# The first tile of a fused attention and MLP kernel in two units of 256 columns, with a rewritten prologue

## The reference

```
k_n = k / (norm(k) + 1e-6)
for t in range(768):
    y[t] = q[t] @ state
    v_old = state.T @ k_n[t]
    state = state + beta[t] * outer(k_n[t], v[t] - v_old)
x = y as (3072, 384)
h = maximum(x @ w_in, 0);  x = (h * h) @ w_out             # w_in 384 x 2048
g = x @ w_gate;  out = (silu(g) * (x @ w_val)) @ w_out2     # 384 x 1536
```

## Time and profile before

| | |
|---|---|
| time, median of 3 runs | 1124.94 us (1123.85 to 1128.55) |
| time of the profiled execution | 1125.86 us |
| its span, first to last instruction | 1124.1 us |
| PE busy | 1002.7 us (89%), 10464 matmuls |
| PE weight loads | 819.2 us (73%) |
| DVE, ACT, POOL busy | 422.8, 289.1, 243.1 us |
| mean granted TensorE clock | 0.983 |
| DMA | 73.83 MB, mean 66 GB/s |

### The profile page before, as it was taken

How to read it: one execution, slowest core, us unless ns; L and a number is a source line. 1 busy time by engine, 2 the same in 40 slices (tenths; PEclk the granted TensorE clock), 3 DMA queues, 4 the chain that set the end, 5 groups by cost and what they waited for, 6 DMA issues and landing times.

```text
span 1124.1 us, 23446 instructions
## 1 busy us (share of the span) xinstructions
PE 1002.7 (89%) x10464; PEld 819.2 (73%) x10464; DVE 422.8 (38%) x662; ACT 289.1 (26%) x553; POOL 243.1 (22%) x351
## 2 busy tenths in 40 slices
PE   2006869979999999999999989999999999999998
PEld 2005747858777777788788868888888888888886
DVE  1562527425354454444425651222222322221322
ACT  2101323313223232223234531121121211211211
POOL 1107706924932860780000000000000000000000
PEclk9999979989999999999999999999999999999999
DMA  7323264143125224213004400010010010100000
GB/s 247 98 76 105 89 181 134 34 118 120 53 56 163 67 71 133 68 36 99 21 2 153 155 29 29 1 57 1 1 57 1 1 57 1 57 1 1 29 1 28
DMA packets 74356, 73.83 MB, mean 66 GB/s; under 512 B 53136, under 2 KB 53264, under 8 KB 74256
## 3 DMA queue, kind: packets, MB, share of 16 engines
q1 hardware_dynamic: 71952, 66.04, 19.8%
q10 hardware_dynamic: 2304, 6.29, 1.6%
HBM read 56.59 MB, written 15.73 MB: 64 GB/s over the span
## 4 chain that ended last, share of the span: by engine, by line
PE 81%; DVE 5%; POOL 5%; DMA 4%; issue 2%; SPq 2%; ACT 1%; DVEq 0%; ACTq 0%; POOLq 0%
PE bank L770 81%; POOL tinv L297 2%; POOL prod L294 2%; DMA k_sq<-in_ky 1%; DMA inv_scratch<-tinv 1%; DVE tinv L297 1%; DVE prod L294 1%; DMA k_prep<-in_kt 1%; SPq L345 1%; PE bank L895 1%; SPq L375 1%; ACT gram L531 1%; DVE h_lo L731 1%; DVE stage L726 0%; DMA inv<-inv_scratch 0%
## 5 line engine op out<-in xcount | busy, mean ns | idle before, releaser
L770 PE MATMUL bank<-x_hi,w_hi 128*128 128x512 f32 x720 | 287.7, 400 | 5.0 <-DVE x_lo L744 3.8
L770 PE MATMUL bank<-x_lo,w_hi 128*128 128x512 f32 x720 | 283.9, 394 | 0.0
L770 PE MATMUL bank<-x_hi,w_lo 128*128 128x512 f32 x720 | 283.5, 394 | 0.0
L770 PE MATMUL bank<-h_hi,w_hi 128*128 128x512 f32 x504 | 202.8, 402 | 1.3 <-DVE h_lo L731 1.3
L770 PE MATMUL bank<-h_lo,w_hi 128*128 128x512 f32 x504 | 196.7, 390 | 0.0
L770 PE MATMUL bank<-h_hi,w_lo 128*128 128x512 f32 x504 | 196.4, 390 | 0.0
L754 DVE TENSOR_TENSOR stage<-bank,stage 128x512 f32<-128x512 f32 x72 | 49.8, 691 | 322.7 <-ACT stage L625 322.7
L770 PEld LDWEIGHTS bank<-x_hi,w_hi 128*128 128x128 f32 x720 | 137.1, 190 | 35.5 <-DVE x_lo L744 4.2
L770 PEld LDWEIGHTS bank<-x_hi,w_lo 128*128 128x128 f32 x720 | 137.3, 191 | 29.2
L770 PEld LDWEIGHTS bank<-x_lo,w_hi 128*128 128x128 f32 x720 | 137.3, 191 | 27.7
L726 DVE TENSOR_TENSOR stage<-stage 128x512 f32<-128x512 f32 x96 | 79.2, 825 | 181.8 <-ACT stage L601 181.6
(11 more groups left out here) (75 smaller groups left out, 604.2 us busy)
## 6 DMA issues: line engine op xcount, KB each, us to landing
w_raw<-in_w SPq DMA_DIRECT2D x12, 576.0 KB, 3.8
k_dim<-in_kt SPq DMA_DIRECT2D x12, 512.0 KB, 4.0
q_dim<-in_qt SPq DMA_DIRECT2D x12, 512.0 KB, 3.6
x1s<-in_w ACTq DMA_DIRECT2D x16, 384.0 KB, 4.0
k_prep<-in_kt SPq DMA_DIRECT2D x11, 512.0 KB, 4.5
k_sq<-in_ky SPq DMA_DIRECT2D x12, 384.0 KB, 3.6
v_tok<-in_vy SPq DMA_DIRECT2D x12, 384.0 KB, 3.6
x_scratch<-x1s SPq DMA_DIRECT2D x18, 256.0 KB, 2.6
```

The costliest lines, as they stand in the source:

```text
L770: return pe.matmul(dst, lhsT, rhs, start=start, stop=stop, **kw)
```

## The change

**Units.** The first MLP's six tiles become seven units (`UNITS`): tile 0 is run as two units of 256 columns, each with all 16 weight blocks, and tiles 1 to 5 as before. Unit 0 needs only chunk 0, so the chain of chunk 1 moves out of the prologue into unit 0, with chunk 2's; chunk 3 is in unit 1. Stages get new slots in all units (`G` at 0 and 10, `lane` at 16).

**Prologue.** Each engine gets a list of its own (`PE_FIRST`, `ACT_FIRST`, `DVE_FIRST`). PE's stages take turns over all eight banks. ACT issues half of tile 0's triangle stores and half of the exchange of its inverses, DVE takes the second bank of `G` 0 and 1, `U` 0, `Z` 0 and `Y` 0 (`SHARED`). `lane` 0 and `solve` 0 stand ahead of the norms of chunks 1 and later; four more staging buffers (`w1_spare`, in memory that `x_hi` and its neighbours use later) hold weight blocks 3 to 6.

**Substitution.** `solve` starts from the factors on the diagonal instead of from ones, so the multiplication of the whole block at its end is gone; the zeroing stands ahead of it. DVE's first block has tiles of its own.

**Elsewhere.** The squares of the keys go from POOL to ACT (`sq`). DVE's square reads relu from `stage` and the product from the PSUM bank, so PE waits for `square_done` instead of `relu_done` before it refills the bank. ACT takes one of the three copies at a unit's end. The split of the second MLP's first input moves ahead of the last nine down matmuls, and the tables for Sqrt and Silu are loaded ahead.

```diff
-    SUB = 2 * (HALF - 1) + 4
+    SUB = 2 * (HALF - 1) + 2
+    UNITS = [(0, 0, T // 2), (0, T // 2, T // 2)] + [(c, 0, T) for c in range(1, NIT)]
...
-        PROLOGUE = [("G", 0), ("root", 0), ("G", 1), ("QK", 0), ("scale", 0), ("G", 2), ("root", 1), ("G", 3),
-                    ("root", 2), ("root", 3), ("w1", 0), ("w1", 1), ("lane", 0), ("solve", 0), ("w1", 2), ("w1", 3),
-                    ("w1", 4), ("U", 0), ("Z", 0), ("lane", 1), ("DZ", 0), ("DS", 0), ("Y", 0), ("scale", 1),
-                    ("KS", 1), ("QK", 1), ("U", 1), ("Z", 1), ("DZ", 1), ("w1", 5), ("Y", 1), ("scale", 2),
-                    ("X", 0, 0), ("X", 0, 1), ("X", 0, 2), ("X", 0, 3)]
-        FIRST_PIECES = 6
+        PE_FIRST = [("G", 0), ("G", 1), ("G", 2), ("G", 3), ("QK", 0), ("U", 0), ("Z", 0), ("DZ", 0), ("Y", 0),
+                    ("DS", 0), ("X", 0, 0), ("X", 0, 1)]
+        ACT_FIRST = [("sq", 0), ("G", 0), ("tri", 0), ("G", 1), ("tri", 1), ("fetch", 1), ("fetch", 2), ("fetch", 3),
+                     ("root", 0), ("w1", 0), ("sq", 1), ("lane", 0), ("fetch", 4), ("fetch", 5), ("fetch", 6),
+                     ("G", 2), ("G", 3), ("w1", 1), ("w1", 2), ("w1", 3), ("w1", 4), ("w1", 5), ("w1", 6), ("fetch", 7),
+                     ("lane", 1), ("inv", 0), ("root", 1), ("U", 0), ("fetch", 8), ("Z", 0), ("sq", 2), ("Y", 0),
+                     ("X", 0, 0), ("X", 0, 1)]
+        DVE_FIRST = [("G", 0), ("root", 0), ("G", 1), ("w1", 0), ("lane", 0), ("solve", 0), ("lane", 1), ("scale", 0),
+                     ("root", 1), ("QK", 0), ("w1", 1), ("U", 0), ("w1", 2), ("w1", 3), ("Z", 0), ("w1", 4), ("DZ", 0),
+                     ("w1", 5), ("Y", 0), ("w1", 6), ("DS", 0), ("X", 0, 0), ("X", 0, 1)]
+        SHARED = [("G", 0), ("G", 1), ("U", 0), ("Z", 0), ("Y", 0)]
...
+            if u == 0:
+                for f, slot in zip(range(7, NF1), (0, 2, 4, 7, 9, 12, 14, 17, 19)):
+                    put(slot, "w1", f)
+                put(1, "scale", 1)
+                put(3, "KS", 1)
+                put(5, "QK", 1)
+                put(6, "U", 1)
+                put(8, "root", 2)
+                put(9, "Z", 1)
+                put(12, "DZ", 1)
+                put(12, "sq", 3)
+                put(15, "Y", 1)
+                put(16, "G", 4)
+                put(17, "root", 3)
+                put(18, "DS", 1)
+                put(20, "X", 0, 2)
+                put(21, "X", 0, 3)
+                put(22, "scale", 2)
+                put(23, "G", 5)
+                put(24, "KS", 2)
+                put(25, "sq", 4)
+                put(26, "QK", 2)
+                put(28, "U", 2)
+                put(29, "lane", 2)
+                put(30, "Z", 2)
+                put(31, "root", 4)
+                put(32, "DZ", 2)
+            elif u == 1:
...
-                for f in range(NF1 - FIRST_PIECES):
-                    put(2 * f + 1, "w1", FIRST_PIECES + f)
-            if c == NIT - 1:
-                for f in range(NF2):
-                    put(2 * f + 3, "w2", f)
+                t, p = u, u + 1
+                n0, n1, p0, p1 = 2 * t, 2 * t + 1, 2 * p, 2 * p + 1
+                if t < NIT:
+                    if p < NIT:
+                        put(0, "G", p0)
+                        put(10, "G", p1)
+                        put(16, "lane", p)
+                    put(2, "sq", n1)
+                    put(4, "root", n1)
+                    put(8, "scale", n1)
+                    chain(n0, dict(KS=2, QK=4, U=5, Z=7, DZ=9, Y=11, DS=12))
+                    chain(n1, dict(KS=14, QK=15, U=17, Z=19, DZ=21, Y=23, DS=24))
...
+        BANKS, BEFORE, holder = {}, {}, {}
+        def take(stage_, numbers):
+            BANKS[stage_] = [banks[b] for b in numbers]
+            BEFORE[stage_] = {holder[b] for b in numbers if b in holder}
+            for b in numbers:
+                holder[b] = stage_
+        turn = 0
+        for one in PE_FIRST:
+            count = 1 if one[0] == "X" else 2
+            take(one, [(5 + turn + i) % 8 for i in range(count)])
+            turn += count
+        FFN_AFTER = {b: holder[b] for b in range(5) if b in holder}
+        turn = 0
...
+        def w1_place(i):
+            if i < RING:
+                return x1s[:, i, :], w1_loaded[i], 1
+            if i < RING + SPARE:
+                return w1_spare[:, i - RING, :], w1_loaded[i], 1
+            k = i - RING - SPARE
+            return x1s[:, k % RING, :], w1_loaded[k % RING], 2 + k // RING
...
+        def solve(eng, t, a, x, products, steps, at):
...
-            then(eng.tensor_tensor(tri[:, :, :], tri[:, :, :], lane_nw[:, :].unsqueeze(1).to_broadcast([P, HALF, HALF]),
+            then(eng.tensor_tensor(a[:, :, :], a[:, :, :], lane_nw[:, :].unsqueeze(1).to_broadcast([P, HALF, HALF]),
                                    ALU.mult))
-            if t > 0:
-                eng.wait_ge(inv_stored, 16 * t)
-            then(eng.memset(tinv[:, :, :], 0.0))
-            then(eng.memset(tinv[:, :, :].rearrange("p s t -> p (s t)")[:, 0:HALF * HALF:HALF + 1], 1.0))
+            then(eng.tensor_copy(diagonal(x), lane_w[:, :]))
             for j in range(HALF - 1):
                 block = [P, j + 1, HALF - 1 - j]
-                share = prod[:, 0:block[1] * block[2]].rearrange("p (c i) -> p c i", i=block[2])
-                then(eng.tensor_tensor(share, tri[:, j:j + 1, j + 1:HALF].to_broadcast(block),
-                                       tinv[:, 0:j + 1, j:j + 1].to_broadcast(block), ALU.mult))
-                below = tinv[:, 0:j + 1, j + 1:HALF]
+                share = products[:, 0:block[1] * block[2]].rearrange("p (c i) -> p c i", i=block[2])
+                then(eng.tensor_tensor(share, a[:, j:j + 1, j + 1:HALF].to_broadcast(block),
+                                       x[:, 0:j + 1, j:j + 1].to_broadcast(block), ALU.mult))
+                below = x[:, 0:j + 1, j + 1:HALF]
                 then(eng.tensor_tensor(below, below, share, ALU.add))
-            then(eng.tensor_tensor(tinv[:, :, :], tinv[:, :, :], lane_w[:, :].unsqueeze(2).to_broadcast([P, HALF, HALF]),
-                                   ALU.mult))
...
+        def first_exchange(eng, i):
+            at = slice(lanes(0, i), lanes(0, i) + HALF)
+            eng.wait_ge(dve_sub_step, SUB)
+            eng.dma_start(inv_dram[0, at, :], first_tinv[at, :, :].rearrange("p s t -> p (s t)")
+                          ).then_inc(first_stored[i], 16)
+            eng.wait_ge(inv_zeroed, 2)
+            eng.wait_ge(first_stored[i], 16)
+            load_blocks(eng, 0, 0, i)
...
             load_k(0)
-            load_prep(1)
             load_ky(0)
-            load_q(0)
-            load_v(0)
             sp.dma_start(beta_sb[:, :, :], beta).then_inc(beta_loaded, 16)
+            store_triangles(sp, 0, 0)
+            store_triangles(sp, 1, 0)
+            load_triangles(0)
             load_prep(2)
-            store_triangles(0)
-            store_triangles(1)
-            load_triangles(0)
-            load_ktok(0)
-            load_k(1)
             load_ky(1)
             load_prep(3)
-            store_triangles(2)
+            load_v(0)
+            load_q(0)
+            load_ktok(0)
+            store_both(2)
+            store_both(3)
+            load_triangles(1)
+            load_prep(4)
+            load_k(1)
+            first_exchange(sp, 0)
...
+            pool.wait_ge(dve_sub_step, SUB)
+            for t in range(1, NIT):
+                if t > 1:
+                    pool.wait_ge(inv_stored, 16 * (t - 1))
+                pool.memset(tinv[:, :, :], 0.0).then_inc(tinv_zeroed, 1)
+                pool.wait_ge(tinv_zeroed, t)
+                solve(pool, t, tri, tinv, prod, sub_step, SUB * (t - 1))
...
-                        slot = stage[:, f % 2, :]
-                        dve.tensor_tensor(slot, slot, slot, ALU.mult).then_inc(square_done, 1)
-                    for stage_ in PLAN[c].get(2 * f, []):
+                        dve.tensor_tensor(stage[:, f % 2, 0:w], stage[:, f % 2, 0:w], up_bank[f % 2][:, 0:w], ALU.mult
+                                          ).then_inc(square_done, 1)
...
-            for c in range(NIT):
-                pe.wait_ge(x_ready, 4 * (c + 1))
+            for u, (c, c0, w) in enumerate(UNITS):
+                at = slice(c0, c0 + w)
+                pe.wait_ge(x_ready, 2 if u == 0 else 4 * (c + 1))
                 for f in range(NF1 + 2):
-                    i = NF1 * c + f
+                    i = NF1 * u + f
                     if f < NF1:
-                        if c == 0:
+                        if u == 0:
                             pe.wait_ge(w1_lo_done, f + 1)
+                        if f < 2:
+                            bank_free(u, f, f)
                         if i >= 2:
-                            pe.wait_ge(relu_done, i - 1)
+                            pe.wait_ge(square_done, i - 1)
                         for kc in range(KC):
                             cols = slice(kc * P, (kc + 1) * P)
```

469 lines of the change are left out of this document (252 added, 217 removed).

## The result

The changed kernel takes 1082.95 us (median of 4 runs, 1082.27 to 1083.66), the kernel before 1125.12 us (4 runs, 1123.85 to 1128.55). The ratio is 0.9614, with a 95% interval of 0.9594 to 0.9633: 42 us faster, where 69 were predicted.

What follows compares the result with a forecast made beforehand. PE was taken as the bound from tile 2 on. Gains of 46.3 (through the short units), 16.7 (tiles 1 to 3) and 6.2 (end) sum to 69.2 off 1125.9; less 0.9 for the median: 1056 us, range 1044 to 1078.

Steps and rivals of the forecast that it cites:

- The start of the substitution: Prologue: an earlier reload of the triangles lets `lane_t` run at 23.2 instead of 44.94, the block done at 49.8.
- From the inverse to the MLP: Prologue: `U` 0 at 56.2, then 15.2 us of stages; the MLP starts at 71.4 instead of 121.3, 49.9 us earlier.
- Unit 0 and 1: The two short units against tile 0: 112 us with stalls, so the middle tiles start at 183.4, 46.3 us earlier.
- the rival of the weight load as a bound: Short units: 256-column matmuls follow after 0.23 us instead of 0.12, giving 1117, or 0.19, giving 1096; chance 0.06.
- I add 7.5 (between 0 and 15): Short units: us added to 104.5 for PE's waits on DVE, ACT and weights and some time at 1.2 GHz.
- Tiles 1 to 3: 90.5 us per tile without stalls; tile 1 gains 11.9, tiles 2 and 3 2.4 each, 16.7 us together.
- The balance "56.3 against 55.9": Middle tiles: 56.3 us of work for the inverse against 55.9 of PE work until `U`; called even, no stall counted.
- The rival of late inverses: Inverses come late in units 2, 3 and 4, 7 us each, giving 1077; chance 0.17.
- The end: Start of the second MLP: the 3.78 us wait and twelve matmuls at 0.43 instead of 0.23 go, 6.2 us gained.
- Edits costed at nothing: Long units: the square from PSUM, ACT's copy and the keys' squares on ACT lie beside PE and cost nothing.

Runs made afterwards that it cites:

- final: lane_first with `lane` 2 at slot 31 instead of 29 of unit 0; 1055.59 us.
- noscrap: The changed kernel without the tile `scrap`, its memset and the two early table loads; 1061.43 us.
- scrap256: The changed kernel with the tile `scrap` at 256 bytes a partition instead of 32; 1063.88 us.
- lane_first: noscrap with `sq` 1 behind `lane` 0 in ACT's list; 1058.27 us.
- lane20: scrap256 with `lane` in the middle units at slot 20 instead of 16; 1094.52 us.

## Why the prediction was wrong, step by step

**The start of the substitution: the path right, the number by luck.** `lane_t` at 23.58 (23.2 predicted), the block done at 50.04 (49.8), by two errors that cancel: the triangles' reload was issued at 14.66, not 16.4, and with it the load of keys at 15.52, not 17.3; that load took 7.3 us, not 5.

**From the inverse to the MLP: right.** `U` 0 at 56.18 (56.2), first MLP matmul at 70.78 (71.4).

**Unit 0 and 1: a term mis-sized.** Short matmuls follow each other after 0.118 us (0.12 predicted, of which the overhead behind 256 columns was the guess), so the rival of the weight load as a bound is out. The rule of the Trainium skill ("TensorE: Matmul & The Clock Gate", Part 3) that a weight load overlaps running matmuls only if it goes to other rows of the array does not fit this trace: 0.118 us from start to start beside loads of 0.19. The step that failed here, the smaller of two, is "I add 7.5 (between 0 and 15)" for stalls: the two units take 120.0 us, 15.5 more than the 104.5 without any. Waits of PE make 8.0 of that, as its waits between 70.8 and 190.8 show:

```profile
PE bank L885 <- DVE h_lo L851: 4.9, 6, 2.6
PE bank L885 <- ACT resid L646: 3.1, 1, 3.1
```

The other 7.5 are largely the clock (0.89 and 0.98 in the windows). The timeline shows it behind the first wait: PE waits 2.58 us, runs one block at 0.12 us from start to start, and behind the next stage the starts lie 0.21 apart, the pace of 256 columns at 1.2 GHz:

```profile
78.09 0.39 PE L885 MATMUL bank<-h_hi,w_hi 128*128 128x256 f32 x1 [2.58 <-DVE h_lo L851]
78.31 0.28 PE L885 MATMUL bank<-h_lo,w_hi 128*128 128x256 f32 x1
78.43 0.28 PE L885 MATMUL bank<-h_hi,w_lo 128*128 128x256 f32 x1
...
82.24 0.41 PE L885 MATMUL bank<-x_hi,w_hi 128*128 128x256 f32 x1
82.45 0.41 PE L885 MATMUL bank<-x_lo,w_hi 128*128 128x256 f32 x1
82.67 0.41 PE L885 MATMUL bank<-x_hi,w_lo 128*128 128x256 f32 x1
```

In final, with about as much waiting (8.4 us) but a granted clock of 1.00, the units take 114.9, so some 5 us hang on the clock. Without their waits the two units take 112.0 us in the changed kernel (clock 0.89 and 0.98), 110.5 in noscrap (0.92, 1.00), 110.3 in scrap256 (0.96, 0.99), 108.9 in lane_first (0.96, 0.99) and 106.5 in final (1.00, 1.00). In the main a higher clock goes with fewer us, but the division is an estimate from traces, not shown by a run that changes the clock alone. I had priced the waits and only mentioned the clock behind them.

**Tiles 1 to 3: right but for the spacing.** 90.3 us each in scrap256 (90.5 predicted), 91.6 with the long spacing. The balance "56.3 against 55.9" was measured as 53.1 against 55.6 for tile 3, 2.5 us of slack, and 1.5 for tile 5: POOL's part took 44.5 us, not 46.9. Tile 1's inverse erred the other way, 50.2 us on POOL where 45 were taken, and was done at 102.5 instead of 97; `U` 2 at 122.8 left room for it. The rival of late inverses didn't occur, and lane20 shows how near it stood.

**The end: the mechanism right, the sum wrong.** The stall and its matmuls at 1.2 GHz are gone: scrap256 gains 5.2 us there (6.2 predicted). But in the changed kernel the whole stretch runs at the longer spacing.

**What failed, and what it weighs.** The step is the one under all terms behind unit 1: that a 512-column matmul keeps the 0.227 us of the earlier trace rows. I took the spacing as a property of the instruction, and compared the diff's tiles for lifetime and size but not for what they displace. The change adds a tile of 32 bytes and moves the weights by 32 against the operand streamed through them. That cost 20.0 us between the spans of the changed kernel and scrap256, by stretches 4.0 in tiles 1 to 3, 1.3 in tile 4 and 14.2 in the last. Of the 7.0 us that are left to the predicted span, the short units make 7.8 and the other stretches together -0.8. With the tile at 256 bytes the same change comes to 1063.9 us, inside the range predicted.

**Edits costed at nothing.** The square from PSUM was a gain of its own: taking it back cost 7.6 us (in the layout with distance 64), about half of it in the short units. The early table loads brought nothing: the first MLP matmul starts at 69.85 without them (noscrap) and at 70.56 with them (scrap256).

**Left open.** Why the distance of two operands in memory matters wasn't tried. Distances of 32, 64, 128 and 224 cost; others, and operands narrower than 4 bytes, weren't measured. The 256-column matmuls varied otherwise (0.1153 us with a distance of 64, 0.1195 with 0), which I can't explain either. That the kernel is faster because of the prologue and the short units together is read from the traces; neither was run alone.

## What to carry to other kernels

When a change adds, resizes or reorders a tile, look at which tiles lie behind it, and compare the distance between the starts of the same matmul in both traces before reading anything else: a fully busy engine can still be 3% slower. In a layout like this one, keep small tiles at sizes of 256 bytes, or behind the operands that PE reads most, and measure the spacing again. A wait of PE is to be priced at more than its length where the windows show a clock below 1.00 behind it; and a slot that the sum calls even wants one run with the slot moved, since here four slots cost 30 us.
